# Chunked recurrence with experts: the opening's exponents completed in PSUM, first scores moved up, units 2 and 3 scored on row halves

## The reference

```python
for t in range(S):
    m_new = np.maximum(f_gate[:, :, t] + m, i_gate[:, :, t])
    f_stab = np.exp(f_gate[:, :, t] + m - m_new)
    i_stab = np.exp(i_gate[:, :, t] - m_new)
    m = m_new
    C = f_stab * C + i_stab * np.einsum('bhd,bhe->bhde', vt, kt)
    n = f_stab * n + i_stab * kt
    h_tilde, nq = C @ qt, n @ qt
    y[:, :, t] = sigmoid(o_gate) * h_tilde / np.maximum(np.abs(nq), 1.0)
...
for e in range(4):
    out += p[:, e:e + 1] * (np.maximum(x @ w1[e], 0) @ w2[e])
```

## Time and profile before

| what | value |
|---|---|
| median of 3 runs | 406.85 us (406.81 to 408.08) |
| profiled execution, own time | 407.32 us |
| its span | 405.4 us |
| PE busy | 400.1 us (99%), 2650 instructions |
| DVE busy | 263.2 us (65%) |
| POOL busy | 194.5 us (48%) |
| ACT busy | 192.7 us (48%) |
| moved by the DMA engines | 54.48 MB, 134 GB/s in the mean |

### The profile page before, as it was taken

How to read it: one execution, slowest core, us unless ns; L and a number is a source line. 1 busy time by engine, 2 the same in 40 slices (tenths; PEclk the granted TensorE clock), 3 DMA queues, 4 the chain that set the end, 5 groups by cost and what they waited for, 6 DMA issues and landing times.

```text
span 405.4 us, 7284 instructions
## 1 busy us (share of the span) xinstructions
PE 400.1 (99%) x2650; PEld 387.3 (96%) x2650; DVE 263.2 (65%) x490; ACT 192.7 (48%) x378; POOL 194.5 (48%) x227
## 2 busy tenths in 40 slices
PE   8999999999999999999999999999999999999997
PEld 8889999999999999999999999889999999999997
DVE  6874886785565465384349893576666666667754
ACT  5575558755355378453125523454454345434420
POOL 5855833665054799733403002567535553556300
PEclk9999999999999999999999999999999999999999
DMA  7989939869152684251024002222112211230002
GB/s 267 289 283 321 412 111 315 314 219 330 43 219 105 213 276 153 97 200 49 2 65 108 0 2 84 86 85 86 44 42 84 86 45 40 84 103 17 0 2 97
DMA packets 18052, 54.48 MB, mean 134 GB/s; under 512 B 2177, under 2 KB 8850, under 8 KB 16866
## 3 DMA queue, kind: packets, MB, share of 16 engines
q1 hardware_dynamic: 17442, 52.63, 38.4%
q10 hardware_dynamic: 576, 1.40, 1.0%
HBM read 50.40 MB, written 2.05 MB: 129 GB/s over the span
## 4 chain that ended last, share of the span: by engine, by line
PE 94%; DMA 2%; DVE 1%; POOL 1%; ACT 1%; issue 0%; SPq 0%; DVEq 0%; POOLq 0%
PE acc_ps L1649 22%; PE hid_ps L1630 21%; PE acc_ps L1720 14%; PE out_ps L1586 5%; PE hid_ps L1720 4%; PE out_ps L1691 2%; PE out_ps L1692 2%; PE out_ps L1694 2%; PE out_ps L1693 2%; PE out_ps L1593 2%; PE score_ps L1530 2%; PE acc_ps L1630 1%; PE add_ps L1691 1%; PE add_ps L1692 1%; PE score_ps L1692 1%; PE add_ps L1694 1%
## 5 line engine op out<-in xcount | busy, mean ns | idle before, releaser
L1173 DVE SCALAR_TENSOR_TENSOR h_lo<-hid_ps,h_hi 128x384 fp32r<-128x384 f32 (+1 forms) x72 | 36.8, 512 | 76.2 <-ACT h_hi L829 75.9
L829 ACT ACTIVATE h_hi<-hid_ps 128x384 fp32r<-128x384 f32 (+1 forms) x72 | 32.8, 456 | 106.9 <-PE hid_ps L1630 106.8
L1649 PE MATMUL acc_ps<-w_hi,h_hi 128*128 128x320 f32 x208 | 66.1, 318 | 0.0
L1649 PE MATMUL acc_ps<-w_hi,h_lo 128*128 128x320 f32 x208 | 64.2, 309 | 0.0
L1649 PE MATMUL acc_ps<-w_lo,h_hi 128*128 128x320 f32 x208 | 64.0, 308 | 0.0
L1630 PE MATMUL hid_ps<-xt_hi,w_hi 128*128 128x384 f32 (+1 forms) x216 | 58.0, 323 | 0.1
L1630 PE MATMUL hid_ps<-xt_hi,w_lo 128*128 128x384 f32 (+1 forms) x216 | 57.6, 320 | 0.3 <-POOL w_lo L632 0.3
L632 POOL TENSOR_TENSOR w_lo<-w_raw,w_hi 128x384 fp32r<-128x384 f32 x40 | 43.5, 1093 | 12.6 <-ACT w_hi L815 12.6
L702 POOL TENSOR_TENSOR w_hi<-w_raw,w_hi 128x640 fp32r<-128x640 f32 x12 | 19.5, 1622 | 51.7 <-ACT w_hi L872 51.7
L606 POOL TENSOR_SCALAR_AFFINE_SELECT dec_w<-dec_w 128x512 f32<-128x512 f32 x22 | 15.2, 692 | 55.5 <-ACT dec_w L794 55.5
L1649 PEld LDWEIGHTS acc_ps<-w_lo,h_hi 128*128 128x128 f32 x208 | 39.2, 189 | 0.1
(11 more groups left out here) (261 smaller groups left out, 996.3 us busy)
## 6 DMA issues: line engine op xcount, KB each, us to landing
w_raw<-in_w_b SPq DMA_DIRECT2D x19, 704.0 KB, 7.3
w_raw<-in_w_s SPq DMA_DIRECT2D x12, 832.0 KB, 4.5
raw<-in_qk_s SPq DMA_DIRECT2D x8, 1024.0 KB
g_all<-g_dram SPq DMA_DIRECT2D x10, 512.0 KB, 6.8
kv<-in_kv_n SPq DMA_DIRECT2D x12, 352.0 KB, 6.5
q_pack<-in_q_p SPq DMA_DIRECT2D x10, 192.0 KB, 6.7
out_y<-y_acc SPq DMA_DIRECT2D x12, 160.0 KB, 1.8
carry<-g_dram SPq DMA_DIRECT2D x30, 60.0 KB
```

Of the source, the lines that this page charges most:

```text
L829: nc.scalar.activation(h_hi[:, M % RING, 0:cols], hid_bank(M)[:, 0:cols], ACT.Relu).then_inc(hid_hi, 1)
L1173: nc.vector.scalar_tensor_tensor(h_lo[:, M % RING, 0:cols], hid_bank(M)[:, 0:cols], 0.0, h_hi[:, M % RING, 0:cols].bitcast(fp32), ALU.max, ...
L1649: last = nc.tensor.matmul(acc_ps[t][:, 0:DM], x, w, start=(f == 0 and i == 0), stop=(f == NF - 1 and i == 2))
```

## The change

- **Exponents of units 0 and 1.** `pick` gets a second plane that gives +1 for j and -1 for the gate sum. `first_sums` writes four parts into `g_parts`: the gate sums' high and low parts (rows 0, 32) and those of `j` (rows 64, 96; the high part by ACT in `high_start`, the low by DVE). `exponents_first` first makes one 512-column product with `g_parts` as weights, which adds what `w_tok` held, and then the four products a half as before, on top of it. The bank then holds the whole exponent, and ACT takes a half in one activation (`first_decays`). The turn of `w`, its copy and one `keep_clock` product go.
- **Order on PE.** `first_scores(0)` stands ahead of the exponents, `move_ends` between the halves; the keys' turn goes behind `outputs(1)`, and `additions(0)` and `(1)` behind `up(0)` and `up(1)`.
- **Order elsewhere.** DVE: `gate_scan(1)` ahead of `gate_x(0)`, `copy_keys` behind `gate_x(1)`. POOL: the head mask first; `split_low(0)`, `unit_sums`, `split_low(1)`, then `weigh_keys`. ACT: `gate_open(0)` behind the exponents. SP: unit 0's scores second, and o's first transfer moved from ACT's queue behind the kv loads.
- **Units 2 and 3.** `paired_scores` makes all scores of a unit at T0, as pairs of 40-row products on the row halves, into `score_ps` and `add_ps`. The zero blocks go; a unit comes in one transfer of 128 rows. `additions` of these units also waits for `p_ready`. Unit 3 begins in slot 7 instead of 6; `keep_heads` of both stands ahead of `gate_x`, and `carry_state` behind the weights' split.

```diff
-T0 = {2: 2, 3: 6, 4: 16, 5: 20, 6: 26, 7: 32, 8: 36, 9: 48, 10: 52, 11: 56}
+T0 = {2: 2, 3: 7, 4: 16, 5: 20, 6: 26, 7: 32, 8: 36, 9: 48, 10: 52, 11: 56}
...
             sp.dma_start(fi_sb, fi_rows).then_inc(gates_in, 16)
+            load_scores(sp, 0)
             sp.dma_start(fi_u[:, :, :], fi_units).then_inc(units_in, 16)
-            load_scores(sp, 0)
             load_scores(sp, 1)
             load_kv(sp, 0)
             load_kv(sp, 1)
+            sp.dma_start(y_acc[:, 0:2, :], o_n[:, 0:2, :]).then_inc(o_in[0], 16)
...
+            def first_decays(k, half):
+                act.wait_ge(e_ready, 2 * k + half + 1)
+                nc.scalar.activation(dec(k, half).rearrange("p h l -> p (h l)"), exp_bank[k, half][:, :], ACT.Exp).then_inc(d_exp, 1)
+            def high_start():
+                gt = gate_tiles[0]
+                act.wait_ge(gt["step"], 2)
+                act.wait_ge(parts_set, 1)
+                nc.scalar.activation(g_parts[64:64 + U0, :], gt["j"][:, :], ACT.Copy).then_inc(j_high, 1)
...
                 nc.vector.tensor_copy(g_parts[0:U0, :], gt["gg"][:, 0, :]).then_inc(g_high, 1)
-                nc.vector.tensor_tensor(gt["w"][:, :], gt["j"][:, :], gt["gg"][:, 0, :], ALU.subtract).then_inc(gt["ready"], 1)
+                dve.wait_ge(j_high, 1)
+                nc.vector.tensor_tensor(g_parts[96:96 + U0, :], gt["j"][:, :], g_parts[64:64 + U0, :].bitcast(fp32),
+                                        ALU.subtract).then_inc(j_low, 1)
...
+                heads = pick[:, 1, k * H + half:(k + 1) * H:2].unsqueeze(2).broadcast_to([128, HALF, L])
+                nc.tensor.matmul(bank[:, :].rearrange("p (a l) -> p a l", a=HALF), g_parts[:, :], heads,
+                                 start=True, stop=False, skip_group_check=True)
                 for a in range(HALF):
                     row = k * H + head_at(k, half, a)
-                    last = nc.tensor.matmul(exp_bank[k, half][:, a * L:(a + 1) * L],
-                                            pick[:, row:row + 1].broadcast_to([128, L]), g_parts[:, :],
-                                            start=True, stop=True)
+                    last = nc.tensor.matmul(bank[:, a * L:(a + 1) * L], pick[:, 0, row:row + 1].broadcast_to([128, L]),
+                                            g_parts[:, :], start=False, stop=True, skip_group_check=True)
...
+            def paired_scores(k):
+                heads = apart[:, kept(k), 0:2 * HALF * L].rearrange("p (t h l) -> p t h l", t=2, h=HALF)
+                pe.wait_ge(qk_in[kept(k)], scores_in(k))
+                pe.wait_ge(p_ready, 2 * k)
+                pe.wait_ge(fresh_ready, k)
+                for a in range(HALF):
+                    for half, bank in ((0, score_ps), (1, score_bank[k, 1])):
+                        rows = slice(64 * half, 64 * half + D)
+                        product = nc.tensor.matmul(bank[:, a * L:(a + 1) * L], heads[rows, 1, a, :], heads[rows, 0, a, :],
+                                                   start=True, stop=True)
+                        if a == HALF - 1:
+                            product.then_inc(s_ready, 1)
```

More of the change, by code:

```diff
@@ L311, in build @@
         score_ps, out_ps, add_ps = bank("score_ps"), bank("out_ps"), bank("add_ps")
-        score_bank = {(0, 0): score_ps, (0, 1): hid_ps[1], (1, 0): acc_ps[0], (1, 1): acc_ps[1]}
+        score_bank = {(0, 0): score_ps, (0, 1): hid_ps[1], (1, 0): acc_ps[0], (1, 1): acc_ps[1],
+                      **{(k, 1): add_ps for k in range(B, NS)}}
         exp_bank = {(0, 0): acc_ps[0], (0, 1): acc_ps[1], (1, 0): out_ps, (1, 1): add_ps}
@@ L721, in _ @@
             unit_steps()
+            split_low(0)
+            unit_sums()
+            split_low(1)
             weigh_keys(0)
             weigh_keys(1)
-            unit_sums()
-            for w in range(FIRST):
+            for w in range(2, FIRST):
                 split_low(w)
@@ L737, in _ @@
                     scale_q(k)
-                if (k := unit_at(M, 6)) is not None and k < NT - B:
+                if (k := unit_at(M, 6)) is not None and NS <= k < NT - B:
                     carry_state(k)
@@ L741, in _ @@
                     split_low(w)
+                if (k := unit_at(M, 6)) is not None and k < NS:
+                    carry_state(k)
                 if M in (59, 61):
@@ L1379, in _ @@
                     subtract_high(k, t)
-                if (k := unit_at(M, 5)) is not None and k < NT - B:
+                if (k := unit_at(M, 5)) is not None and NS <= k < NT - B:
                     keep_heads(k)
@@ L1532, in scores @@
+            def scores(k, half):
+                pe.wait_ge(p_ready, 2 * k + half)
+                pe.wait_ge(sub_done, 2 * (k - NS) + 2)
+                for a in range(HALF):
+                    h = half * HALF + a
+                    last = nc.tensor.matmul(score_ps[:, a * L:(a + 1) * L], split_qk[:, kept(k), 1, h, :],
+                                            split_qk[:, kept(k), 0, h, :], start=True, stop=True)
                 last.then_inc(s_ready, 1)
@@ L1808 @@
     w = _np.concatenate([w1.reshape(NE, NF, 128, 384), inputs["moe_w2"].reshape(NE, NF, 128, DM)], axis=3)
-    apart = _np.zeros((NS, KA, 2, HALF, L), q.dtype)
-    apart[:, 0:D, 0], apart[:, 0:D, 1] = q[:NS, :, 0::2], k[:NS, :, 0::2]
-    apart[:, 64:KA, 0], apart[:, 64:KA, 1] = k[:NS, :, 1::2], q[:NS, :, 1::2]
+    apart = _np.zeros((NS - B, 128, 2, HALF, L), q.dtype)
+    for half in range(2):
+        rows, heads = slice(64 * half, 64 * half + D), slice(half * HALF, (half + 1) * HALF)
+        apart[:, rows, 0], apart[:, rows, 1] = q[B:NS, :, heads], k[B:NS, :, heads]
     first = _np.zeros((B, 128, 2, HALF, L), q.dtype)
```

125 lines of the change are left out of this document (48 added, 77 removed).

## The result

The change made the kernel slower: 415.64 us, median of six runs (413.41, 408.67, 417.55, 413.94, 417.34, 417.34), against 407.44 for six runs of the kernel before (406.81 to 408.08). The ratio is 1.0117 with a 95% interval of 1.0089 to 1.0144; it leaves out the three runs at 417, which the comparison takes for disturbed, and which the experiments show to be the kernel's own doing. The forecast was 405.8, the range 404.7 to 407.2.

A forecast was written before the change was run, and what follows sets the result against it. PE was taken to bound the kernel: its issued work plus its waits. Terms of -0.3, +1.2, -1.2, -0.9 and +0.2 sum to -1.0 us, forecasting 405.8 us, range 404.7 to 407.2.

The forecast's parts named there:

- term 1: Opening up to `up(0)`: quicker exponents, POOL steps and unit 1's x start `up(0)` earlier, -0.3 us.
- Term 2: Additions of units 0 and 1 leave PE's idle time for the dense part behind `up(0)` and `up(1)`, +1.2 us.
- Term 3: PE's two waits for `w_lo` in the `up`s go, as `g_all`'s chain starts earlier and PE arrives later, -1.2 us.
- rival of the returning waits: ACT hands POOL high halves late, reopening a `w_lo` wait in `up(10)`, or unit 3's turn costs more; 406.85 us, chance 0.14.
- Term 4: Scores of units 2 and 3 as pairs on row halves take 1.25 us a unit instead of 1.72, -0.9 us.
- cheap rival: Row halves switch at no cost and POOL is quicker in the opening: -2.0 us in all, 404.8 us, chance 0.13.
- late transfer: Opening: unit 0's scores land late and hold PE up ahead of the exponents; up to +0.7 us, 407.5, chance 0.10.
- Term 5: Unit 3's x, turned in slot 13, comes slightly late for `up(16)` in slot 14, +0.2 us.
- The clock rival: PE's clock falls back in the sparse gap before `up(0)`, costing 1.9 us: +0.9 in all, 407.7 us, chance 0.07.

The follow-up runs named there:

- e4: e1 with GpSimd's gate steps for units 2 to 11 put ahead of its first weight block; 407.87 us, ratio 1.0016.
- e2: Kernel before with units 2 and 3 on row halves, unit 3 a slot later, kept heads and state steps reordered, old opening; 406.69 us, ratio 0.9974.
- e7: e4 with the additions of units 0 and 1 back ahead of `up(0)` and what they need put early; 406.72 us, ratio 0.9990.
- e3: Kernel before with only the new opening, units 2 and 3 scored as before; 414.15 us.
- e9: Kernel before with only the selector's tile `pick` twice as wide, 64 bytes a partition more; 410.34 us.
- e1: Changed kernel with GpSimd waiting in slot 48 until VectorE has done the first subtraction on unit 10; 409.18 us, ratio 1.0044.
- e11: Changed kernel with an unused tile of 192 bytes a partition behind the selector, no wait in slot 48; 409.45 us.
- e12: e7 without its wait in slot 48, with an unused tile of 192 bytes a partition behind the selector; 406.87 us, ratio 0.9989.
- e5: Changed kernel with a fill of 16 numbers on VectorE ahead of unit 10's first subtraction in slot 49; 416.91 us.
- e8: e4 without the wait in slot 48; 409.89 us.
- e13: e10 with its scratch tile 1,024 bytes a partition instead of 880; 417.58 us.
- e6: Kernel before with a fill of 8 numbers on GpSimd ahead of the mask in slot 48; 407.12 us.
- e10: Changed kernel with three fills of 220 numbers on VectorE ahead of slot 49's first subtraction, in an 880-byte scratch tile; 408.84 us.
- e14: Kernel before with the selector's tile 128 bytes a partition wider; 407.29 us, ratio 0.9999.

## Why the prediction was wrong

Two steps failed. The sum has no term behind unit 3's turn in slot 14, so it puts everything later at nothing; there the wider selector moved tiles, and slots 40 to 58 cost 4.63 us: 2.84 are PE's wait for `h_lo`, and 1.7 the clock, at half for 3.4 us. And term 1 gave the moved scan the duration it had beside other neighbours. Term by term:

**Term 1, the opening (-0.3): right but for one duration.** With the scan unhindered, warm to `up(0)` is 12.13 (e4) against 12.39, -0.26, and unit 1's x is done at 16.47 where 16.6 was forecast. The step that failed is "the scan stands ahead of unit 0's gating and waits for POOL: 12.9 to 13.6". I took 0.74 us from the earlier trace rows without asking what GpSimd would do beside it, though I wrote two parts later that it now splits weights first. The block begins with the scan and costs it 0.8 (1.23 us against 0.42 in e4); the term was +0.58. The further +0.92 in the start is not the change's: the warming products took 4.57 us before and 5.49 after, but 5.49 in e2 as well, which has the old opening.

**Term 2, the additions (+1.2): right.** 3.29 became 4.54, and e7, which puts them back, has 3.27 again and a median 1.15 under e4's.

**Term 3, the waits for `w_lo` (-1.2): right in size, the reason not shown.** The two are gone: third kind of product 0.48 after the first in both `up`s, where it was 1.21 and 1.01. The reason given was an earlier `g_all` against a later PE. The sixteen traces agree that the waits go with this distance (6.6 us and more with them, 6.0 and less without). But the earlier scan does not set it alone: the load of `g_all` was issued 4.8 us after the last store in e3, 3.4 before and 2.0 in e2, and e9, the old order with a wider tile, shows no listed wait and is 0.89 us shorter up to slot 24. One trace a kernel cannot say what the change does to it. A small wait is left in a later `up` (at 46.2 us in e4): its third kind stands 0.70 after its first, 0.22 too late, and GpSimd's block ended only as the `w_lo` product began. That is the rival of the returning waits, in small.

**Term 4, row halves (-0.9): a little less.** From the first score product to the next work, the two units took 3.09 us before and 2.19 after; but the first pair also stands 0.09 us further behind the product ahead of it, so the term is -0.72. The switch back cost about 0.2 as charged; the cheap rival is out. So is the late transfer: unit 0's scores (issued at 1.2) landed 3.5 us after their issue, and PE never waited for them. The 3.09 us are less than the 3.44 that the prediction's 0.86 a half gives: two of the four halves took 0.68 to the next start.

**Term 5, unit 3 a slot later (+0.2): about right.** In `up(16)` the third kind of product stands 0.81 after the first instead of 0.48, so the wait for x that was foreseen costs 0.33. With it, the 0.22 of term 3's last wait and terms 3 and 4 at -1.98, the stretch to slot 24 comes to -1.4, and it measured -1.41 in e4.

**The clock rival** named the place, the gap before `up(0)`, and the cause. By the clocks it happened in half of e1's runs and five of e11's six, at 1.1 us in e1's trace and 1.35 in e11's. I gave it 0.07 and argued that PE had stood before without harm; the gap became 1.00 + 0.67 us, since the lost scan widened it.

**What no term held** is slot 49. The wider selector looked free. Nor did the prediction look at where VectorE and GpSimd already shared the ports with no slack: in the trace before GpSimd runs 23 operations from 147.05 to 170.0 us without a pause, and four of `subtract_high`'s operations, with two SBUF inputs each, fall among them.

The best versions are e2 (406.69, ratio 0.9974), then e7 and e12 (0.9990, 0.9989). They beat the kernel before by 0.3% and 0.1%, little but outside the intervals; e7 and e12, which have the new opening too, show no gain over e2.

## What to carry to other kernels

When GpSimd runs a row of operations without a pause, give VectorE's two-input operations beside it a wait of GpSimd's own to slip into, as e1 does: here it cost nothing that shows (e7 with it 406.72, e12 without but padded 406.87) and took 6 us off the median. When a change slows a stretch that it does not touch, cut both timelines at the same events first, and look there for one instruction far above its median; and test the layout by widening one tile in the old kernel, with enough runs to see a second group of times, before explaining anything by the order of the work. A duration read from the trace holds only with the neighbour it had.

## What the runs showed that was not expected

- The loser of the VectorE and GpSimd lock can be held for a whole row of instructions: 6.96 us for a 1.2 us operation in four traces (after, e5, e8, e9), and 6.13 in e13, where it came 0.8 later.
- Whether that happens depended on a shift of SBUF tiles by 64 bytes a partition; 128 and 256 never showed it. The 64-byte layouts are also a little slower without it: from the 289th to the 433rd down product 52.93 to 52.95 us (e1, e3, e4, e7) against 52.80 (before, e2, e6, e10, e11, e12). But e14, shifted by 128, has 52.93 too, so 128 is not quite the old layout.
- With PE idle for 2.8 us the clock fell to half in all five profiled runs that have it, but for 3.4 us (after, e8, e9) or 10.2 us (e5, e13); two runs of e9 had times that fit the idle time and a clock of 1.0. What decides the length no run shows.
